# Scores for 64 keys at a time, keys times values in the state's layout, and loads moved to ACT's queue

## What is computed

```python
# per batch and head, for t in 0..767 (ar, ai: normalised a_re, a_im)
S_re, S_im = ar*S_re - ai*S_im + outer(k[t], v[t]), ar*S_im + ai*S_re
y[t] = q[t] @ S_re                       # 48 x 48 state
# x: (4, 768, 384), heads side by side
u  = x + (x^T @ U @ V)^T                 # rank 32 over the tokens
x2 = u + relu(u @ w_ch1) @ w_ch2         # 384 -> 1536 -> 384
theta = x2 @ w_theta
x3 = x2 + w_tok_r @ (x2*cos(theta)) + w_tok_i @ (x2*sin(theta))
out = x3 + relu(x3 @ w_ch)
```

## Time and profile before

| | us |
|---|---|
| median of 3 runs | 780.65 (779.03 to 780.88) |
| the profiled execution | 780.54 |
| its span, first to last instruction | 778.8 |
| TensorE matmuls busy | 710.3 (91%) |
| DVE busy | 503.9 (65%) |
| ACT busy | 417.3 (54%) |
| mean granted TensorE clock | 0.991 |

### The profile page before, as it was taken

How to read it: one execution, slowest core, us unless ns; L and a number is a source line. 1 busy time by engine, 2 the same in 40 slices (tenths; PEclk the granted TensorE clock), 3 DMA queues, 4 the chain that set the end, 5 groups by cost and what they waited for, 6 DMA issues and landing times.

```text
span 778.8 us, 13125 instructions
## 1 busy us (share of the span) xinstructions
PE 710.3 (91%) x4944; PEld 683.4 (88%) x4944; DVE 503.9 (65%) x918; ACT 417.3 (54%) x913; POOL 220.8 (28%) x175
## 2 busy tenths in 40 slices
PE   0028999999999999999999999999999999999998
PEld 0027879999999979999999979999999879999998
DVE  6978858699458758597458747597448832224634
ACT  8875757665464636673464637674463621223531
POOL 0003582433430053222530053223440000113350
PEclk9998999999999999999999999999999999999999
DMA  9645540010246850010136950010136840000121
GB/s 325 201 110 144 146 176 5 1 42 1 61 120 192 218 203 21 1 42 0 61 104 193 235 203 21 0 42 1 42 103 183 227 144 37 1 1 1 42 61 61
DMA packets 42734, 73.45 MB, mean 94 GB/s; under 512 B 8784, under 2 KB 23376, under 8 KB 42672
## 3 DMA queue, kind: packets, MB, share of 16 engines
q1 hardware_dynamic: 42384, 72.23, 31.6%
q10 hardware_dynamic: 288, 0.39, 0.2%
HBM read 48.96 MB, written 4.72 MB: 69 GB/s over the span
## 4 chain that ended last, share of the span: by engine, by line
PE 83%; DVE 7%; ACT 4%; DMA 3%; issue 2%; SPq 1%; DVEq 0%; ACTq 0%
PE bank L1181 80%; DMA region<-qk 2%; PE bank L1351 1%; DVE stream L924 1%; PE bank L1262 1%; PE bank L1191 1%; PE bank L1221 1%; DMA region<-stream 1%; DVE logr L862 1%; DVE ST L954 1%; DVE qk L937 1%; DVE phasor L913 0%; DVE phasor L904 0%; SPq L333 0%; ACT scale L626 0%
## 5 line engine op out<-in xcount | busy, mean ns | idle before, releaser
L1181 PE MATMUL bank<-uT,w_sb 128*128 128x384 f32 x864 | 167.8, 342 | 0.0
L1181 PE MATMUL bank<-hT,w_sb 128*128 128x384 f32 x864 | 165.0, 337 | 0.0
L1181 PE MATMUL bank<-tok,z 128*128 128x384 f32 x864 | 158.7, 337 | 0.6 <-issue 0.2
L1181 PEld LDWEIGHTS bank<-uT,w_sb 128*128 128x128 f32 x864 | 153.1, 192 | 1.5 <-ACT uT L691 1.2
L1181 PEld LDWEIGHTS bank<-hT,w_sb 128*128 128x128 f32 x864 | 151.2, 188 | 0.3 <-DVE hT L1083 0.3
L1181 PEld LDWEIGHTS bank<-tok,z 128*128 128x128 f32 x864 | 149.3, 188 | 1.8 <-POOL tok L511 1.8
L1083 DVE SCALAR_TENSOR_TENSOR hT<-bank,hT 128x384 fp32r<-128x384 f32 x96 | 52.8, 550 | 72.0 <-ACT hT L683 71.7
L683 ACT ACTIVATE hT<-bank 128x384 fp32r<-128x384 f32 x96 | 46.5, 484 | 83.3 <-PE bank L1181 83.1
L511 POOL TENSOR_TENSOR tok<-tok_low,tok 128x768 fp32r<-128x768 f32 x20 | 38.1, 1907 | 86.8 <-ACT tok L713 86.8
L1191 PE MATMUL bank<-ident,stream 128*128 128x128 f32 x72 | 11.3, 297 | 48.6 <-DVE stream L937 48.6
L519 POOL TENSOR_TENSOR x_sb<-uT 128x384 f32<-128x384 f32 x24 | 25.1, 1074 | 102.2 <-DVE uT L1077 69.2
(11 more groups left out here) (147 smaller groups left out, 1310.7 us busy)
## 6 DMA issues: line engine op xcount, KB each, us to landing
stream<-in_qk SPq DMA_DIRECT2D x24, 384.0 KB, 3.8
tok_low<-in_w_tok SPq DMA_DIRECT2D x20, 384.0 KB, 3.5
stream<-in_a SPq DMA_DIRECT2D x19, 384.0 KB, 4.4
scale<-in_w_tok SPq DMA_DIRECT2D x16, 384.0 KB, 4.2
w_raw<-in_w SPq DMA_DIRECT2D x12, 384.0 KB, 7.6
region<-qk SPq DMA_DIRECT2D x16, 256.0 KB, 3.6
region<-stream SPq DMA_DIRECT2D x15, 256.0 KB, 3.1
stream<-in_v SPq DMA_DIRECT2D x16, 192.0 KB, 4.9
```

The source lines that it names most:

```text
L1181: return t.matmul(o, lhsT, rhs, start=start, stop=stop, is_transpose=turned)
```

## The change

Five things are changed.

- Scores are computed for 64 keys at a time. Per head there are two matmuls, one for keys 0 to 63 against all 128 queries, one for keys 64 to 127 against queries 64 to 127 alone (the quarter in which all keys come after the queries is left at the zero that a memset put there, or at old finite numbers, and masked). Even heads put their first 64 keys on partitions 0 to 63 and their last on 64 to 127; odd heads the other way round. The mask has a second, exchanged version for odd heads, `both_tri`, and `values` takes odd heads' v from `v_odd`, in which the two halves of each 128 tokens are exchanged. The host provides it as an input `v_turned`, 192 columns wide.
- `keys_values` has `Kn` as weights and v moved, and writes 96 partitions of bank 2 in the state's layout. `turn_state` and ACT's copy to `KV` are gone.
- `next_state` waits for s_kv, and before it overwrites the state, for the end of values(c). `keys_values` waits for the sum of the chunk before.
- Within a batch `load_qk(c+3)` and `load_v(c+2)` are issued by ACT, between keys_to_sbuf(c) and decays(c+2). The loads at the start of a batch stay with SP. Every `load_v` is two DMAs.
- At the start DVE has one memset more and builds the exchanged mask in two copies.

```diff
+        both_tri = sb("both_tri", [P, 2, P])
+        tri = both_tri[:, 0, :]
+        v_turned_sb = sb("v_turned_sb", [P, 2, PAIRS * HD])
-        KV = tA[:, :].rearrange("p (j d) -> p j d", j=PAIRS)
+        v_odd = (stream[:, 10 * D + 2 * H * P:10 * D + 2 * H * P + PAIRS * HD], v_turned_sb[:, 0, :], v_turned_sb[:, 1, :])
-        s_v_in = [sem(f"s_v_in{i}", C // 3, 16) for i in range(3)]
+        s_v_in = [sem(f"s_v_in{i}", C // 3, 32) for i in range(3)]
...
                 sp.dma_start(v_in[c % 3], v[b, c * P:(c + 1) * P, :]).then_inc(s_v_in[c % 3].sem, 16)
+                sp.dma_start(v_odd[c % 3], v_turned[b, c * P:(c + 1) * P, :]).then_inc(s_v_in[c % 3].sem, 16)
...
                 for c in range(C - 1):
-                    if c + 3 < C and (c >= 1 or b == 0):
-                        load_qk(b, c + 3)
-                    if c >= 1 and c + 2 < C:
-                        load_v(b, c + 2)
...
+            def load_qk(b, c):          # on ACT
+                if c >= 2:
+                    act.wait_ge(s_Q.sem, s_Q.at(b, c - 1))
+                act.dma_start(qk_in[c % 2], ...).then_inc(s_qk_in[c % 2].sem, 16)
+            def load_v(b, c):           # on ACT
+                if c >= 3:
+                    act.wait_ge(s_yt.sem, s_yt.at(b, c - 2))
+                act.dma_start(v_in[c % 3], ...).then_inc(s_v_in[c % 3].sem, 16)
+                act.dma_start(v_odd[c % 3], ...).then_inc(s_v_in[c % 3].sem, 16)
             def attention(b, c):        # on ACT
                 if c + 1 < C and (b or c):
                     keys_to_sbuf(b, c)
+                if c + 3 < C and (c >= 1 or b == 0):
+                    load_qk(b, c + 3)
+                if c >= 1 and c + 2 < C:
+                    load_v(b, c + 2)
                 if 1 <= c < C - 2 and (b or c >= 2):
                     decays(b, c + 2)
                 if c >= 1:
                     rows_of_x(b, c - 1)
-                if c + 1 < C:
-                    act.wait_ge(s_kv.sem, s_kv.at(b, c + 1))
-                    ...
-                    a.activation(KV[0:112, :, :], bank[4][0:112, 0:D]...).then_inc(s_kv_sb.sem, 1)
...
-                d.tensor_tensor(ST[:, 4 * i:4 * i + 4, :], heads(score_bank[i][:, :]),
-                                tri[:, :].unsqueeze(1).broadcast_to([P, 4, P]), ALU.mult)\
+                d.tensor_tensor(ST[:, 4 * i:4 * i + 4, :].rearrange("p (j e) t -> p j e t", e=2),
+                                score_bank[i][:, :].rearrange("p (j e t) -> p j e t", e=2, t=P),
+                                both_tri[:, :, :].unsqueeze(1).broadcast_to([P, 2, 2, P]), ALU.mult)\
...
-                dve.wait_ge(s_kv_t.sem, s_kv_t.at(b, c + 1))
+                dve.wait_ge(s_kv.sem, s_kv.at(b, c + 1))
...
+                if c >= 1:
+                    dve.wait_ge(s_yt.sem, s_yt.at(b, c + 1))
                 d.tensor_tensor(now, total, gain_rows...)
...
-            d.memset(bank[4][:, :], 0.0).then_inc(s_zero.sem, 1)
+            for i in range(2):
+                d.memset(score_bank[i][:, :], 0.0).then_inc(s_zero.sem, 1)
+            dve.wait_ge(s_const.sem, CONSTANTS)
+            d.tensor_copy(both_tri[0:MID, 1, :], tri[MID:P, :])
+            d.tensor_copy(both_tri[MID:P, 1, :], tri[0:MID, :]).then_inc(s_tri.sem, 1)
...
-                for h in range(4):
-                    ins = mm(heads(score_bank[i][:, :])[:, h, :], rows[c % 3][0:2 * HD, 4 * i + h, 1, :],
-                             rows[c % 3][0:2 * HD, 4 * i + h, 0, :])
+                for pair in range(2):
+                    for late in range(2):
+                        for odd in range(2):
+                            h, lo, t0 = 2 * pair + odd, MID * (odd ^ late), MID * late
+                            ins = mm(heads(score_bank[i][lo:lo + MID, :])[:, h, t0:P],
+                                     rows[c % 3][0:2 * HD, 4 * i + h, 1, t0:t0 + MID],
+                                     rows[c % 3][0:2 * HD, 4 * i + h, 0, t0:P])
...
                 for h in range(H):
-                    lo = 64 * (h % 2)
-                    ins = mm(bank[4][lo:lo + HD, 2 * HD * (h // 2):2 * HD * (h // 2 + 1)],
-                             v_in[c % 3][:, h * HD:(h + 1) * HD], Kn[:, h, :])
+                    ins = mm(bank[2][0:2 * HD, h * HD:(h + 1) * HD], Kn[:, h, :], v_in[c % 3][:, h * HD:(h + 1) * HD])
...
-                ins = mm(o, v_in[c % 3][:, h * HD:(h + 1) * HD], ST[:, h, :], stop=c == 0)
+                of = v_odd[c % 3][:, h // 2 * HD:(h // 2 + 1) * HD] if h % 2 else v_in[c % 3][:, h * HD:(h + 1) * HD]
+                ins = mm(o, of, ST[:, h, :], stop=c == 0)
```

More of the change, by code:

```diff
@@ L27, in at, with token_mixer_program @@
         return b * (self.per_batch * self.unit) + (n + self.ahead) * self.unit
-def token_mixer_program(nc, v, qk_rows, a_rows, U, V, w1, w2, w_tc, w_tok, out):
+def token_mixer_program(nc, v, v_turned, qk_rows, a_rows, U, V, w1, w2, w_tc, w_tok, out):
     B, S, D = v.shape
@@ L42, in token_mixer_program @@
     MID = P // 2
+    ZEROED = 3
     G = D // P
@@ L654, in rows_of_x @@
                              ACT.Copy).then_inc(s_x.sem, 1)
+            def load_qk(b, c):
+                if c >= 2:
+                    act.wait_ge(s_Q.sem, s_Q.at(b, c - 1))
+                act.dma_start(qk_in[c % 2], qk_rows[b, c * P:(c + 1) * P, :].rearrange("p (i j t) -> p i j t", i=G, j=2))\
+                    .then_inc(s_qk_in[c % 2].sem, 16)
+            def load_v(b, c):
+                if c >= 3:
+                    act.wait_ge(s_yt.sem, s_yt.at(b, c - 2))
+                act.dma_start(v_in[c % 3], v[b, c * P:(c + 1) * P, :]).then_inc(s_v_in[c % 3].sem, 16)
+                act.dma_start(v_odd[c % 3], v_turned[b, c * P:(c + 1) * P, :]).then_inc(s_v_in[c % 3].sem, 16)
             def attention(b, c):
@@ L963, in next_state @@
                 now, total = state[0:2 * HD, :, :], state_sum[0:2 * HD, :, :]
-                kv = bank[2][0:2 * HD, :].rearrange("p (j e d) -> p j e d", e=2, d=64)[:, :, :, 0:HD]
-                dve.wait_ge(s_kv_t.sem, s_kv_t.at(b, c + 1))
+                kv = pairs(bank[2][0:2 * HD, 0:D].rearrange("p (h d) -> p h d", h=H))
+                dve.wait_ge(s_kv.sem, s_kv.at(b, c + 1))
                 if c == 0:
@@ L1206, in keys_values @@
                 if c >= 1:
-                    pe.wait_ge(s_kv_sb.sem, s_kv_sb.at(b, c))
+                    pe.wait_ge(s_sum.sem, s_sum.at(b, c))
                 elif b:
-                    pe.wait_ge(s_out.sem, s_out.at(b - 1, KD + 1))
+                    pe.wait_ge(s_out.sem, s_out.at(b - 1, KD + 2))
                 for h in range(H):
-                    lo = 64 * (h % 2)
-                    ins = mm(bank[4][lo:lo + HD, 2 * HD * (h // 2):2 * HD * (h // 2 + 1)],
-                             v_in[c % 3][:, h * HD:(h + 1) * HD], Kn[:, h, :])
+                    ins = mm(bank[2][0:2 * HD, h * HD:(h + 1) * HD], Kn[:, h, :], v_in[c % 3][:, h * HD:(h + 1) * HD])
                 ins.then_inc(s_kv.sem, 1)
-            def turn_state(b, c):
-                pe.wait_ge(s_kv_sb.sem, s_kv_sb.at(b, c + 1))
-                if c >= 1:
-                    pe.wait_ge(s_sum.sem, s_sum.at(b, c))
-                for j in range(PAIRS):
-                    ins = t.transpose(heads(bank[2][0:2 * HD, :])[:, j, 0:112], KV[0:112, j, :], ident[0:112, 0:112])
-                ins.then_inc(s_kv_t.sem, 1)
             def values(b, c):
@@ L1253, in attention @@
                 values(b, c)
-                if c + 1 < C:
-                    turn_state(b, c)
             def outputs(b, c):
@@ L1449, in _ @@
             pe.wait_ge(s_const.sem, CONSTANTS)
-            pe.wait_ge(s_zero.sem, 2)
+            pe.wait_ge(s_zero.sem, ZEROED)
             key_columns(0, 0)
@@ L1472, in features_first, with odd_heads_halves_turned @@
         return np.concatenate([wide, rest], axis=1)
+    def odd_heads_halves_turned(x):
+        b, h, s, d = x.shape
+        odd = x.transpose(0, 2, 1, 3)[:, :, 1::2, :].reshape(b, s // P, 2, P // 2, -1)
+        return np.ascontiguousarray(odd[:, :, ::-1]).reshape(b, s, -1)
     def shape(x):
         return x.shape[0], x.shape[2], -1
-    arrays = {"v": tokens_first(inputs["v"])}
+    arrays = {"v": tokens_first(inputs["v"]), "v_turned": odd_heads_halves_turned(inputs["v"])}
     qk = np.stack([features_first(inputs[n]) for n in ("q", "k")], axis=3)
```

11 lines of the change are left out of this document (2 added, 9 removed).

## The result

| | before | after |
|---|---|---|
| median, us | 779.73 (10 runs, 777.23 to 781.64) | 789.41 (10 runs, 782.97 to 791.33) |
| ratio to before | | 1.0113, 95% interval 1.0090 to 1.0136 |
| profiled execution, its span | 780.54, 778.8 | 789.52, 787.8 |
| mean granted TensorE clock | 0.991 | 0.985 |
| attention stage of batch 1, 2, 3, 4 | 57.4, 42.9, 42.8, 44.0 | 53.9, 44.7, 49.6, 44.6 |

The kernel is slower by about 9.7 us, which is clear of the noise. The forecast was 781.5, with 779 to 784 as its own range. The time lies outside that range and just inside the outer one, 776 to 790, near rival (a)'s 787.5. All ratios in this document are taken over fast executions alone, and of all those measured only two of e9's, 790.99 and 791.41 us, were slow (without them its median is 781.5 us). A stage is counted here from its first key_columns to the first matmul of the work behind it.

What follows compares the result with a forecast made beforehand. TensorE's own work was taken as the bound, with a chain ACT, DVE, SP, DMA delivering rows close behind. 780.54 + 0.4 (TensorE) + 3 x 0.1 (waits) + 0.3 (first batch) = 781.5 us; range 779 to 784, outer 776 to 790.

Steps and rivals of the forecast that it cites:

- rival (a): ACT's queue becomes the bound: late issues and landing of 5.2 to 6.4 us, about +7, 787.5 us; chance 0.23.
- TensorE's steps: Attention chunks 0 to 4: scores -0.45, keys_values +0.67, turn_state -0.38, split/whole changes +0.27, sum +0.11 us; four batches +0.4.
- Rival (b): Scores: halves overlap in matmuls but not weight loads, so scores stays at 1.79 or 1.92; 790 us; chance 0.12.
- rival (c): keys_values costs less than its weight load suggests, say 60 ns a matmul: -8 us, 773.5 us; chance 0.20.
- ACT's delay: ACT's queue: three issues of 0.65 us ahead of decays make rows(3) issue 1.3 us later.
- The step that failed: ACT's queue: loads issued from 425.6 are through by 433; rows(3) lands in 4.5 us, scores(3) 0.5 later.
- The exchanged v: DMA in attention: 96 KB a chunk beside 960, 10% more, the reason not to take a landing of 3.4 us.
- The first batch: First attention stage: shorter scores(0) against ACT's issues and decays, +0.3 us taken, bounds -1 and +2.
- The clock: Behind the third batch's stage: six microseconds at mean granted clock 0.72, 1.7 us that may come or go.

Runs made afterwards that it cites:

- e9: Changed kernel with its loads on SP's queue and 512-byte transfers from ACT in the places of its loads: 783.04 us.
- e6: Changed kernel without the exchanged v (exchange of halves left out), loads still on ACT's queue: 782.33 us.
- e7: Changed kernel without the exchanged v (exchange of halves left out), loads back on SP's queue: 775.01 us.
- e4: Kernel before with only keys_values in the state's layout, no turn_state and no copy to KV: 779.16 us.
- e5: Kernel before with only scores in blocks of 64 keys, exchanged v and mask with it, loads on SP: 786.76 us.
- e8: Kernel before with only scores in blocks of 64 keys, loads on SP, no exchanged v: 777.81 us.
- e1: Changed kernel with load_qk and load_v back in SP's queue, everything else as changed: 782.75 us.
- e2: Kernel before with only load_qk and load_v moved to ACT's queue, no exchanged v: 793.20 us.
- e3: Changed kernel with ACT's loads issued behind decays(c+2) instead of ahead of it: 783.23 us.

## Why the prediction was right and wrong

**TensorE's steps were right.** In an undisturbed chunk, from the timelines and above:

| step | before | after | change | predicted |
|---|---|---|---|---|
| keys_values | 0.69 | 1.41 | +0.72 | +0.67 |
| turn_state | 0.42 | 0 | -0.42 | -0.38 |
| key_columns, scores, outputs, values, with the changes between split and whole array | 4.83 | 4.67 | -0.16 | -0.45 + 0.27 = -0.18 |
| sum | 5.94 | 6.08 | +0.14 | +0.11 |

Scores' last matmul starts 1.34 us after its first, so both halves of the array load and multiply at once, as predicted. Rival (b) fell by that, and rival (c), a cheaper keys_values, by its 1.41. But these steps were not what decided the time.

**ACT's delay was right in size.** Its three issues were taken at 0.65 us each and show 0.35 to 0.47. DVE stands idle for 1.15 us before it scales chunk 3, and the last copy of rows(3) is issued at 433.07 for 431.97, 1.1 us later for the 1.3 foretold. But e9 shows that such a delay costs nothing that can be measured.

**The step that failed** is in the part on ACT's queue: "those are issued from 425.6 on and are through by 433". The times are about right (425.71, and the last landing at 433.8). Two things were wrong in what was made of them. The first is that rows(2) was not considered at all. The loads are issued at 425.71, in the middle of rows(2)'s four copies, which I could have placed from the same trace: they are on SP's queue from 425.01 on, and their last landing of 3.5 us ends only 0.6 us ahead of scores(2). I followed rows(3), the wait that was there, and not the rows that had been on time. In after that landing took 7.3 us, and TensorE waited for it and then ran at 1.2 GHz, 7.65 us in all in the third batch. The second is the landing that I took for rows(3), 4.5 us, between the 3.3 of a quiet queue and the 5.0 of a pair of queues in the first batch that carried little. It was 6.0, 7.4 and 6.7 in the three later batches, in two of them above the 5.2 to 6.4 that I had as the upper bound. The bound came from a queue with loads ahead in it. Nothing in that row could bound a case where 670 KB flow beside.

**The exchanged v** was only "the reason not to take the clean 3.4", 10% more bytes. It costs 7.1 to 7.7 us (e6, e7). A share of bytes is no price: the rows have some tenths of a microsecond of slack in a chunk, and what comes on top makes TensorE wait.

**Rival (a)** forecast 787.5 and was the nearest number, by another mechanism. Its landing stayed long, as it said, but ACT was no bound: its 1.3 us for late issue is what e9 refutes. That the time lies within 776 to 790 is thus luck. The upper bound was set by rival (b), with (a) below it, and neither came true; no term of the prediction had what cost the time. The 0.40 given to a slower kernel came from the same two rivals.

**The first batch** was mis-sized: +0.3 was taken, with -1 as the bound, and -3.5 came (-4.0 in e7). In before, values(1) there waits for its masks, and the clock falls:

```profile
69.92 0.67 PE L1181 MATMUL bank<-ST,stream 128*48 128x128 f32 x4 [3.63 <-DVE ST L954]
```

The clock is at its lower level for 6.8 us from 68.7 on, which costs another 3.4. The prediction says that after the start only waits for rows written from qk come to more than a microsecond; the list has this one too:

```profile
PE bank L1181 <- DVE ST L954: 3.8, 2, 3.6
```

It is missing in after, and 0.96 in e4 without a fall of the clock, while e5 and e8 have it with 4.12 and the fall. So it is the state's new path that removes it, not the scores. How it does so is less plain. In after the masks come earlier (66.6 us for 69.1), partly because DVE no longer waits for turn_state. In e4 they come no earlier (70.2); there TensorE comes later, with keys_values(1) at 68.6 for 65.4. DVE's operations ahead of the masks are also long in one kernel and short in another (L911 and L913 1.80 and 2.04 us in before, their counterparts 0.36 and 0.56 in after). What makes them long was not tried.

**The clock** was taken at 1.7 us either way. It came to 5.1 + 3.4 in the later batches. In these traces the waits ahead of scores that were followed by a fall are the long ones, so a first microsecond of waiting and a third one do not cost the same.

## What to carry to other kernels

Before moving transfers to a second queue, write down which transfers stand behind which in the first: a queue that issues urgent copies ahead of loads gives them a priority, and a second queue takes it away. Check the transfers that are just in time, not only those that are late: subtract landing from use for each, here 0.6 us for rows(2). Price added transfers by where they flow: the same 96 KB a chunk cost 7.7 us beside the rows, 2.3 with most of them fetched before the stage, and nothing that showed once the rows also went first.

## What the runs showed of the hardware

- Two queues together: a copy of 128 KB landed 3.5 to 3.6 us after its issue with loads behind it on its own queue (before, rows(2)), and in 5.6 to 7.3 with 670 KB issued beside it from ACT (after).
- In the later stages, seven waits of TensorE of 1.94 to 2.86 us ahead of scores were followed by 3.4 to 10.2 us at 1.2 GHz, in after and in e1, e2, e3, e5 and e6. One of 1.99 in e5 and one of 1.90 in e8 were not, nor were waits of 0.8 to 1.5 in several kernels. The stretches of 3.4 us behind the stages came in none (e4) to all four (after) of the batches, after idle times that are alike in all of them (0.89 us ahead of the first matmul that reads Z, in the later batches), so I can't say what decides there.
- The spread between runs of a kernel went with it: e3's ran from 779.4 to 788.0 us, e4's, whose profile has no such stretch before the last microseconds, from 777.9 to 780.7.
- Two halves of the array with 64 weight columns each multiply and load at once for float32: 32 matmuls of scores in 1.34 us, 42 ns each (half of them with 128 moved columns, half with 64), for 112 ns with 128 columns on the whole array.
- The halves don't keep the program's order between them: values issues all four matmuls of an even head before those of the odd one, yet in after the odd head's first starts at 428.79, 0.01 us behind the even head's first and 0.24 us ahead of its third (429.04).
